# Third pair's loads ahead of the scale's values, and the looks through weights, values and gate spread over the first five pairs

## The reference

```python
def phi(x):                                  # batch 4, heads 8, rows 576, head size 64, features 128
    proj = einsum('bhsd,df->bhsf', x, w_phi)
    proj = proj - max(abs(proj), axis=-1)
    return concatenate([exp(proj), exp(-proj)], axis=-1)
q_p, k_p = phi(q), phi(k)
kv = einsum('bhsf,bhsd->bhfd', k_p, v);  z = sum(k_p, axis=2)
x = (q_p @ kv) / (q_p . z + 1e-6)            # then laid out as (N, D)

P = exp(x @ w_gate - max)                    # 8 experts; 8 rounds of row and column scaling
x = sum over e of P[:, e] * relu(x @ w1[e]) @ w2[e]          # F = 1024, every row, every expert

# second mixture: cosine logits against expert_emb / tau; each row goes to its best expert alone
out[row] = gate[row] * relu(x[row] @ w1b[e]) @ w2b[e]
```

## Time and profile before

| what | value |
|---|---|
| median of 3 runs | 2067.83 us |
| the profiled execution's own time | 2064.49 us |
| its span | 2062.7 us |
| PE busy | 2032.3 us, 99% of the span |
| DVE busy | 1008.4 us, 49% |
| ACT busy | 696.3 us, 34% |
| POOL busy | 174.8 us, 8%, of it nearly all in the attention and at the end |
| mean granted clock of PE | 0.995 |
| DMA, size of one issue | q or k of a pair 288 KB each; v of a pair 2 x 128 and 2 x 16 KB; half of the values 2304 KB; w1 or w2 of an expert 2048 KB |

### The profile page before, as it was taken

The page is one execution under the profiler, slowest core; times in us unless marked ns, Lnnn a source line. Parts: engine busy times, 40 slices in busy tenths (PEclk is TensorE's granted clock), DMA queues, the critical chain, the costliest instruction groups (busy, mean ns, idle before and its releaser), DMA issues.

```text
span 2062.7 us, 31690 instructions
## 1 busy us (share of the span) xinstructions
PE 2032.3 (99%) x12658; PEld 1206.2 (58%) x12658; DVE 1008.4 (49%) x1606; ACT 696.3 (34%) x1372; POOL 174.8 (8%) x179
## 2 busy tenths in 40 slices
PE   7999999999999999999999999999999999899998
PEld 6888755555555555555555555555555565566775
DVE  6888855544444444444444444444444433644433
ACT  6666533333333333232333333333323332222221
POOL 0753300000000000000000000000000000211110
PEclk9999999999999999999999999999999999899999
DMA  7222111221122112212211221221122240731600
GB/s 215 65 63 65 47 63 61 82 82 41 41 82 82 42 55 99 93 41 82 83 41 42 82 82 42 93 103 51 41 82 82 82 184 21 277 142 45 272 26 8
DMA packets 93247, 169.38 MB, mean 82 GB/s; under 512 B 60454, under 2 KB 60582, under 8 KB 89776
## 3 DMA queue, kind: packets, MB, share of 16 engines
q1 hardware_dynamic: 89104, 157.92, 21.7%
q0 software_dynamic: 4000, 9.45, 1.4%
HBM read 126.19 MB, written 44.83 MB: 83 GB/s over the span
## 4 chain that ended last, share of the span: by engine, by line
PE 96%; DVE 1%; DMA 1%; SPq 1%; issue 0%; ACT 0%; POOL 0%; POOLq 0%; DVEq 0%
PE ps L668 36%; PE ps L687 36%; PE ps L869 6%; PE ps L853 4%; PE ps L612 3%; PE ps L627 3%; PE ps L855 2%; PE ps L591 2%; PE ps L600 1%; DMA arena<-in_k_dram 1%; PE ps L576 1%; PE ps L732 1%; PE ps L824 1%; PE ps L702 0%; SPq L360 0%
## 5 line engine op out<-in xcount | busy, mean ns | idle before, releaser
L668 PE MATMUL ps<-arena 128*128 128x384 f16 x4608 | 774.4, 326 | 0.4 <-issue 0.4
L687 PE MATMUL ps<-arena 128*128 128x512 f16 x3456 | 769.6, 379 | 0.0
L668 PEld LDWEIGHTS ps<-arena 128*128 128x128 f16 x4608 | 450.4, 98 | 312.3 <-issue 0.8
L687 PEld LDWEIGHTS ps<-arena 128*128 128x128 f16 x3456 | 338.1, 98 | 391.1 <-DVE arena L1164 0.2
L973 ACT ACTIVATE arena<-ps 128x384 f32<-128x384 f32 x384 | 188.5, 491 | 1019.5 <-PE ps L668 1015.5
L1268 DVE TENSOR_TENSOR arena<-arena 128x384 f16<-128x384 f32 x384 | 214.0, 557 | 312.8 <-ACT arena L977 311.7
L1323 DVE SCALAR_TENSOR_TENSOR arena<-ps,wt,arena 128x512 f32<-128x512 f32 x126 | 94.5, 750 | 435.2 <-PE ps L687 435.0
L977 ACT ACTIVATE arena<-ps 128x384 f16<-128x384 f32 x384 | 186.0, 484 | 0.0
L1148 DVE TENSOR_REDUCE wg<-arena 128x1 f32<-128x1024 f32 x128 | 154.8, 1211 | 28.6 <-DMA arena<-in_moe_w_dram 28.5
L1164 DVE SCALAR_TENSOR_TENSOR arena<-arena,wsc 128x1024 f16<-128x1024 f32 x124 | 158.3, 1277 | 0.8 <-ACT arena L939 0.6
L939 ACT ACTIVATE arena<-arena,wsc 128x1024 f16<-128x1024 f32 x124 | 142.6, 1150 | 1.9 <-DVE wsc L1095 1.9
(11 more groups left out here) (203 smaller groups left out, 1184.8 us busy)
## 6 DMA issues: line engine op xcount, KB each, us to landing
arena<-in_moe_w_dram SPq DMA_DIRECT2D x32, 2048.0 KB, 8.8
split_weights<-arena SPq DMA_DIRECT2D x16, 2048.0 KB, 7.4
arena<-split_weights SPq DMA_DIRECT2D x8, 4096.0 KB
arena<-in_q_dram SPq DMA_DIRECT2D x16, 288.0 KB, 3.6
arena<-in_k_dram SPq DMA_DIRECT2D x16, 288.0 KB, 3.9
arena<-in_v_dram SPq DMA_DIRECT2D x2, 2304.0 KB, 12.6
x_rows<-arena SPq DMA_DIRECT2D x18, 256.0 KB, 2.4
arena<-in_v_dram SPq DMA_DIRECT2D x32, 128.0 KB, 2.3
```

The source lines that it names most:

```text
L668: last = pe.matmul(o, ring[:, slot, sw, FF * c + 128 * j:FF * c + 128 * j + 128], xT[:, sx, c, BLK * blk:BLK * blk + BLK], start=(n == 0), ...
L687: last = pe.matmul(ps[:, Y_PS + tt, :], hbuf[:, blk % 2, sh, f, 128 * tt:128 * tt + 128], ring[:, slot, 2 + sw, D * f:D * f + D], start=(n ...
```

## The change

It moves and re-splits the preparatory work of the first pairs.

- SP: the weights' load comes ahead of the second v; q and k of pair 2 come directly behind it (after the wait for pair 0's transposes); the values are loaded as 3/8 and 5/8 instead of two halves.
- ACT sums three pieces of the values in pair 1 and four in pair 2; DVE does the eighth in pair 2 (`last_squares`).
- DVE looks through the weights' quarters 0 and 1 in group 0 of pair 1, 2 in group 2 of pair 1, 3 in group 0 of pair 3. The weights' scale moves from pair 2 to pair 4, the look through the gate from pair 1 to pair 4.
- POOL does the values' all-reduce first, the weights' one behind the quotients of pair 0, the gate's one behind those of pair 3.

```diff
--- before.py
+++ after.py
@@ -202,7 +202,8 @@
         X_LAST = xT[:, :, H // 2 - 1, N - S:N]
 
         VSUMS, VW = 8, N * D // 128 // 8
-        VSUM_AT = {1: (0, 1, 2, 3), 2: (4, 5, 6, 7)}
+        LOOK_AT = {(1, 0): 1, (1, 2): 2, (3, 0): 3}
+        VSUM_AT = {1: (0, 1, 2), 2: (3, 4, 5, 6)}
 
         def due(value):
 
@@ -243,7 +244,7 @@
         xsplit_done = sem("xsplit_done")
         last_scaled, last_hi, last_split = sem("last_scaled"), sem("last_hi"), sem("last_split")
 
-        vsum_done, vall_in = sem("vsum_done"), pair_of("vall_in")
+        vsum_done, vlast_done, vall_in = sem("vsum_done"), sem("vlast_done"), pair_of("vall_in")
         vmax_done, vall_done, vscale_chain = sem("vmax_done"), sem("vall_done"), sem("vscale_chain")
         gmax_done, gall_done, gscale_done = sem("gmax_done"), sem("gall_done"), sem("gscale_done")
         gate_cut = sem("gate_cut")
@@ -365,7 +366,7 @@
                 sp.dma_start(raw.rearrange("p (c f) -> p c f", c=src.shape[1]), src).then_inc(raw_in, 16)
 
             def load_values(half):
-                cols = slice(half * N * D // 256, (half + 1) * N * D // 256)
+                cols = (slice(0, 3 * VW), slice(3 * VW, VSUMS * VW))[half]
                 sp.dma_start(vall[:, cols], vall_v[:, cols]).then_inc(vall_in[half], 16)
 
             load_qk(0, 0)
@@ -375,16 +376,19 @@
             load_values(0)
             sp.wait_ge(vone_done, 5)
             load_v(0, 0)
+            load_raw(0, w1a_v[0])
+            sp.wait_ge(turned, GP)
+            load_qk(2, 0)
             load_v(1, 1)
-            load_raw(0, w1a_v[0])
             load_values(1)
             sp.dma_start(gate_raw[:, :, :], w_gate.rearrange("(c p) e -> p c e", p=128)).then_inc(small_in, 16)
             sp.dma_start(emb_sb[:, :], emb).then_inc(small_in, 16)
             sp.dma_start(tau_sb[:, :], tau.partition_broadcast(128)).then_inc(small_in, 16)
 
             def later_pairs(i, u):
-                sp.wait_ge(turned, GP * (i - 1))
-                load_qk(i, u)
+                if i > 2:
+                    sp.wait_ge(turned, GP * (i - 1))
+                    load_qk(i, u)
                 sp.wait_ge(kv_done, i - 1)
                 load_v(i, u)
 
@@ -476,9 +480,7 @@
                 pool.tensor_tensor(ring[:, 0, 2 * n + 1, cols], raw[:, cols], ring[:, 0, 2 * n, cols], ALU.subtract)\
                     .then_inc(wlo_done, 1)
 
-            across(wm[:, :], wg[:, :], RMAX, wmax_done, 1, wall_done)
             across(vm[:, 0:1], vm[:, 1:2], RMAX, vmax_done, 1, vall_done)
-            across(gsc[:, 0:1], gsc[:, 1:2], RMAX, gmax_done, 1, gall_done)
             def cut_x(b):
                 for hp in range(H // 2):
                     i = b * (H // 2) + hp
@@ -499,10 +501,14 @@
                     pool.tensor_tensor(xT[:, 1, hp, cols], xq[:, u, :], xT[:, 0, hp, cols], ALU.subtract)\
                         .then_inc(xsplit_done, 1)
                     pool.wait_ge(xsplit_done, i + 1)
+                    if i == 0:
+                        across(wm[:, :], wg[:, :], RMAX, wmax_done, 1, wall_done)
                     if i in SPLIT:
                         split_weights(0, SPLIT[i])
 
-            for b in range(B):
+            cut_x(0)
+            across(gsc[:, 0:1], gsc[:, 1:2], RMAX, gmax_done, 1, gall_done)
+            for b in range(1, B):
                 cut_x(b)
             across(wm[:, :], wg[:, :], RMAX, wmax_done, 2, wall_done)
             across(sk[:, 0:1], sk[:, 1:2], RMAX, sk_red, 1, sk_all)
@@ -954,7 +960,7 @@
 
             def values_sums(pieces):
                 for k in pieces:
-                    act.wait_ge(vall_in[2 * k // VSUMS], 16)
+                    act.wait_ge(vall_in[k // 3 and 1], 16)
                     piece = vall[:, VW * k:VW * k + VW]
                     act.activation(piece, piece, ACT.Square, accum_out=vmp[:, k:k + 1]).then_inc(vsum_done, 1)
 
@@ -1168,28 +1174,39 @@
                 for par in range(2):
                     for u, g, up, nxt, prev in groups(c, par, first, last and par == 1):
                         features(u, up)
-                        if first and par == 1 and g == 2:
+                        if isinstance(c, int) and (2 * c + par, g) == (4, 1):
                             dve.wait_ge(small_in, 16 * 3)
                             dve.tensor_reduce(gsc[:, 1:2], gate_raw[:, :, :].rearrange("p c e -> p (c e)"), AX, ALU.max,
                                               apply_absolute_value=True).then_inc(gmax_done, 1)
                         if not first:
                             invert(2 * c + par - 2, g, par)
+                        if first and par == 1 and g == 0:
+                            largest(0, 0)
                         if prev is not None:
                             side(g, prev, 1 - par)
 
-                        if first and par == 1:
-                            for k in ((0,), (1, 2), (3,))[g]:
-                                largest(0, k)
+                        if isinstance(c, int) and (2 * c + par, g) in LOOK_AT:
+                            largest(0, LOOK_AT[2 * c + par, g])
                         if isinstance(c, int):
+                            if 2 * c + par == 2 and g == 0:
+                                last_squares()
                             if 2 * c + par == 2 and g == 1:
                                 values_bound()
-                            if 2 * c + par == 2 and g == 2:
+                            if 2 * c + par == 4 and g == 0:
                                 weight_scale(0, winv[:, 0:1])
                             if 2 * c + par == 3 and g == 0:
                                 values_scale()
 
+            def last_squares():
+                dve.wait_ge(vall_in[1], 16)
+                for k in range(VSUMS - 1, VSUMS):
+                    piece = vall[:, VW * k:VW * k + VW]
+                    dve.tensor_tensor_reduce(piece, piece, piece, 1.0, 0.0, ALU.mult, ALU.add, vmp[:, k:k + 1])\
+                        .then_inc(vlast_done, 1)
+
             def values_bound():
-                dve.wait_ge(vsum_done, VSUMS)
+                dve.wait_ge(vlast_done, 1)
+                dve.wait_ge(vsum_done, VSUMS - 1)
                 dve.tensor_reduce(vm[:, 1:2], vmp[:, :], AX, ALU.max).then_inc(vmax_done, 1)
 
             def values_scale():
```

## The result

The changed kernel took 2077.66 us as the median of 8 runs (2072.51 to 2080.26), the kernel before 2067.27 us (8 runs, 2062.35 to 2069.18). The ratio is 1.0051, interval 1.0041 to 1.0060: 10.5 us slower, 8.5 to 12.4. The forecast time was 2080.5 us, 2.8 above the measured one.

What follows compares the result with a forecast made beforehand. TensorE bounds the kernel (96% of the chain of waits), but GpSimd's four extra configuration changes delay it: +12.4 and 2.0 for the clock make +14.4. Forecast 2080.5 us, between 2078.9 and 2082.2; range 2076 to 2086 at 0.72.

Steps and rivals of the forecast that it cites:

- +14.4: Whole kernel: 12.4 us later at pair 7's second quotient product, plus 2.0 for TensorE's clock.
- k earlier: Loads: third pair's k lands at 21 to 29 us against 31.4 needed; gain 2.6 us, bounds 0 and 2.7.
- Squares on VectorE: Pair 2: the eighth square sum on VectorE takes 1.4 us, bounds 0.7 and 2.7; hidden, taken as 0.
- Pair 3: Pair 3: the look ahead of the values' scale delays TensorE 1.0 us and denominators 0.2, +1.2 in all.
- Without GpSimd -1.3: First pairs: k's -2.6, the look's +1.2 and the weight scale's +0.15 sum to about -1.3 us.
- Changes outward: GpSimd, out of the weights' and gate's all-reduces: 7.34 us each, bounds 7.3 and 8.1.
- Changes inward: GpSimd, into the weights' and gate's all-reduces: 7.34 us each, bounds 0 and 8.1.
- Rival 1: Inward configuration changes are cheap: at 3 us each the shift is +3.7, time 2070 to 2074; chance 0.12.
- Chain and slack: GpSimd's queue from the values' scale on: stall of 3.8 us in pair 4, pair 7's second quotient product 12.4 later.
- a1+a2+b1+b2-17.0: Shift at pair 7 in us: inward changes a1, a2 plus outward b1, b2, less 17.0; forecast 12.4.
- Clock: TensorE after the stalls: granted clock at 0.50 costs 1.0 to 3.5 us, 2.0 taken after pair 7, nothing in pair 4.

Runs made afterwards that it cites:

- two one-block kernels with an earlier look: Changed kernel with all three all-reduces in one block; fourth look in pair 2: 2062.91 us, ratio 0.9991; all looks in pair 1: 2063.89 us, ratio 0.9986.
- one-block run: Changed kernel with all three all-reduces in one block ahead of the first quotients, gate's look in pair 2: 2073.28 us, ratio 1.0032.

## Why the prediction was right

The direction, the place and the mechanism held: four extra configuration changes, stalls in pairs 4 and 7 before the second quotient product, TensorE's clock down behind the second. The sum was +14.4; measured were 10.5 (8.5 to 12.4), so the sum was too high by 3.9. By its own steps:

- *k earlier.* Right. k landed at 24.1 (issued at 13.80, 10.3 to landing), in the range of 21 to 29 that I gave, and its transposes start at 28.46. The DMA instruction held SP for 5.19 there.
- *Squares on VectorE.* 1.34 and 0.08 for the read-out, I had 1.4; hidden, as said.
- *Pair 3.* It took 1.13 more than before; I had 1.2.
- *Without GpSimd -1.3.* No run shows it alone. The two one-block kernels with an earlier look, which don't pay the 1.2 of pair 3, came to 1.8 to 2.9 below.
- *Changes outward.* 7.04 and 7.35; I had 7.34 for each, 0.3 too much in all.
- *Changes inward.* The step that was mis-sized. I took the outward row for a price of which the trace gave only the bounds 0 and 8.1; it is 5.88 and 5.89 (5.7 to 6.1 in seven profiles). That is 2.9 of the 3.9 us between sum and result. Rival 1 had the right direction and too low a price (3). My argument against it, that both kinds bear the same pair of config instructions, overlooked that the earlier trace rows have them at 8 and 83 ns.
- *Chain and slack.* With the measured prices the formula a1+a2+b1+b2-17.0 gives 9.2, and 2.0 for the clock 11.2. A cut with a quarter took 11.56 per round instead of 11.65, 0.3 less over three. That leaves 10.9, which is what the profile shows with the early start taken out; the last 0.4 is within the interval.
- *Clock.* I had 2.0 behind pair 7; L633 took 1.94 longer, and the projections behind it were at their normal 0.94. In pair 4 the clock also fell (L633 took 3.34). By the chain that costs nothing at the end, since pair 7 waits for GpSimd anyway; no run tests this alone.

One gap in the forecast did no harm here: I listed the needs of pairs 4 to 8 and left out that of pair 3, which the changed order still met (quotient of pair 0 at 51.8, wanted at 57.3). The same gap made the next expectation, that of the one-block run, wrong by 9 us. In pair 3 the forecast was right by the order of the block and not by my reasoning.

The Trainium skill (GPSIMD Engine Reference, section Instruction dispatch) gives approximately 6 us, 5.95 measured from the configuration instruction on, for the load at the first call to a freshly loaded kernel. The trace agrees on the way into the all-reduce, with 5.88 and 5.89. On the way out the profiles of this case have 6.9 to 7.6, and there the measurement decides.

## What to carry to other kernels

Count the changes of kind in GpSimd's stream, not its busy time: an engine at 8% was the bound in pairs 4 and 7 here, because each all-reduce moved in among ordinary work brought two changes, some 13 us in which it did nothing. In this kernel the two versions with one early block had the lowest medians, so all-reduces are best kept in one block, and the last input of that block has to be ready early enough for one change outward before the first result is wanted. When a queue in program order is lengthened, list every later wait on it with its due time, the first one too; the loss is what exceeds the slack, which two additions share.

## What was not expected of the hardware

The inward change takes 5.7 to 6.1 us and the outward one 6.9 to 7.6, behind config instructions of one name that take 5 to 11 and 82 to 83 ns.

Executions of one program differ in when TensorE becomes fast at the start. The clock records of the twelve profiles begin near 14 us in two, near 17.5 in three and between 21.5 and 23 in seven, each time where the products become shorter; between the first and the last lie some 2.8 us of the whole time.

In the attention stage a stall of 2.1 to 2.9 us was followed by a granted clock of 0.50 in four cases and left it at 1.00 in four, the kernel before's 2.72 among them; one profile (only GpSimd's order) has both, 2.77 with and 2.27 without. Near 1740 us even a stall of 1.11 was followed by 0.50, in seven profiles of twelve, at a price of 1.7 us in the one shown above.
